# A recurrent attention with two feed-forward layers: four edits to the order of work around the turns of a half batch

## What is computed

```
for t in range(S):
    cur = einsum('bhd,bhe->bhde', u * k[t], v[t])
    y[t] = einsum('bhd,bhde->bhe', r[t], state + cur)
    state = w[t][:, None] * state + einsum('bhd,bhe->bhde', k[t], v[t])
```

## Time and profile before

| | us |
|---|---|
| median of three runs | 777.52 |
| lowest, highest | 776.89, 780.5 |
| the profiled execution's own time | 781.25 |
| its span, first to last instruction | 779.5 |
| TensorE busy | 733.1 (94%) |
| VectorE busy | 475.7 (61%) |
| ScalarE busy | 365.6 (47%) |
| GpSimd busy | 392.9 (50%) |
| mean granted TensorE clock | 0.987 |

### The profile page before, as it was taken

How to read it: one execution, slowest core, us unless ns; L and a number is a source line. 1 busy time by engine, 2 the same in 40 slices (tenths; PEclk the granted TensorE clock), 3 DMA queues, 4 the chain that set the end, 5 groups by cost and what they waited for, 6 DMA issues and landing times.

```text
span 779.5 us, 17757 instructions
## 1 busy us (share of the span) xinstructions
PE 733.1 (94%) x6779; PEld 516.6 (66%) x6779; DVE 475.7 (61%) x967; ACT 365.6 (47%) x735; POOL 392.9 (50%) x372
## 2 busy tenths in 40 slices
PE   4699999999989999999999999998999999999995
PEld 4466656656655665665666666556688878788783
DVE  6998898779666878776787864645333333333331
ACT  3652577656655756746756665542122212212210
POOL 5445488769668869778777876252111111111111
PEclk9998999999999999999999999999999999999998
DMA  9835636365364653645545247994699866766763
GB/s 341 324 150 185 209 132 244 105 241 174 131 238 179 234 215 121 233 165 172 201 142 187 82 162 243 341 345 158 225 383 395 294 245 214 254 237 219 265 222 116
DMA packets 42694, 170.04 MB, mean 218 GB/s; under 512 B 5198, under 2 KB 13136, under 8 KB 37104
## 3 DMA queue, kind: packets, MB, share of 16 engines
q1 hardware_dynamic: 30160, 108.18, 39.1%
q10 hardware_dynamic: 8928, 50.51, 18.5%
q0 software_dynamic: 3520, 10.17, 3.3%
HBM read 132.30 MB, written 37.33 MB: 218 GB/s over the span
## 4 chain that ended last, share of the span: by engine, by line
PE 60%; POOL 9%; DMA 9%; DVE 6%; issue 6%; ACT 3%; SPq 1%; ACTq 0%; POOLq 0%; DVEq 0%
PE bank L1733 5%; PE bank L1876 5%; PE bank L1878 5%; PE bank L1877 5%; PE bank L1735 4%; PE bank L1734 4%; PE bank L1724 4%; PE bank L1722 4%; PE bank L1721 4%; PE bank L1842 4%; PE bank L1844 4%; PE bank L1843 4%; DMA arena<-w_exp_dram 3%; POOL act_buf L606 3%; DMA route_rows<-xrow,pos 2%
## 5 line engine op out<-in xcount | busy, mean ns | idle before, releaser
L606 POOL TENSOR_TENSOR act_buf<-act_buf 128x384 f16<-128x384 f32 x128 | 120.2, 939 | 139.8 <-ACT act_buf L809 138.8
L1291 DVE SCALAR_TENSOR_TENSOR act_buf<-neg,slope,bank 128x384 f32<-128x384 f32 x128 | 77.7, 607 | 92.1 <-ACT neg L802 91.4
L692 POOL DMA_INDIRECT out_dram<-neg,dest x28 | 27.5, 984 | 201.7 <-DVE neg L1560 194.2
L1733 PE MATMUL bank<-arena,act_buf 128*128 128x392 f16 x384 | 127.2, 331 | 1.6 <-ACT xrow L765 1.4
L1721 PE MATMUL bank<-xh,arena 128*128 128x384 f16 x384 | 125.5, 327 | 2.2 <-DVE xl L1093 1.5
L1734 PE MATMUL bank<-arena,act_buf 128*128 128x392 f16 x384 | 127.1, 331 | 0.0
L1735 PE MATMUL bank<-arena,act_buf 128*128 128x392 f16 x384 | 127.0, 331 | 0.0
L1722 PE MATMUL bank<-xl,arena 128*128 128x384 f16 x384 | 125.3, 327 | 0.0
L1842 PE MATMUL bank<-shared,arena 128*128 128x128 f16 x672 | 114.1, 219 | 1.9 <-DVE shared L1486 1.7
L1844 PE MATMUL bank<-shared,arena 128*128 128x128 f16 x672 | 114.1, 219 | 0.0
L1843 PE MATMUL bank<-shared,arena 128*128 128x128 f16 x672 | 114.1, 219 | 0.0
(11 more groups left out here) (185 smaller groups left out, 1563.9 us busy)
## 6 DMA issues: line engine op xcount, KB each, us to landing
arena<-expert_split ACTq DMA_DIRECT2D x28, 1536.0 KB, 7.5
arena<-w_exp_dram SPq DMA_DIRECT2D x32, 768.0 KB, 6.3
expert_split<-arena SPq DMA_DIRECT2D x32, 768.0 KB, 4.7
arena<-expert_split SPq DMA_DIRECT2D x9, 1536.0 KB, 9.2
arena<-rk_in_dram SPq DMA_DIRECT2D x24, 512.0 KB, 6.0
arena<-rk_tok_dram SPq DMA_DIRECT2D x24, 384.0 KB, 3.3
arena<-w_dram SPq DMA_DIRECT2D x24, 256.0 KB, 6.8
shared<-route_rows ACTq DMA_DIRECT2D x31, 197.0 KB, 2.5
```

What stands on the lines that cost most here:

```text
L606: pool.tensor_tensor(gl[:, f % 4, :], gf[:, f % 4, :], gh[:, f % 4, :], ALU.subtract).then_inc(gl_done, 1)
L1733: pe.matmul(at, gh[:, f % 4, ts], woh[:, f, :], start=(f == 0), stop=False)
```

## The change

- VectorE: `y_rows` of the third chunk moves from turn 13 to the end of turn 12, ahead of line 1291 of block 13.
- GpSimd: the third indirect DMA of `scatter` moves from turn 15 to turn 14, and all three now stand ahead of the turn's other work.
- SyncE: `load_w2(0)` moves from the end of the third half's transfers into the middle of the fourth's, ahead of `store_hu(j + 1)` and `load_hu(j + 3)`.
- The multiplication for the tokens between (`inverses`, line 1053) moves for the 20 chunks from the fifth on (m > 3) from VectorE to GpSimd (`inverses_even`), directly ahead of `decayed_k`, and waits for `odd_done` there.

```diff
@@ -457,6 +457,13 @@
             load_rk(1, 0, 2)
             load_tok(1, 0, 2)
 
+            def load_w2(e):
+
+                for i in range(2):
+                    sp.wait_ge(split_out[i], UP + 16 * (2 * e + 2))
+                sp.dma_start(arena[:, w2_at(e):w2_at(e) + 2 * UNIT], wsplit[e][:, 2 * UNIT:4 * UNIT]
+                             ).then_inc(w2_in[e], 16)
+
             def middle(g, j):
                 b, half = g // 2 + 1, g % 2
                 if b < B:
@@ -474,6 +481,9 @@
                 if b < B:
                     load_tok(b, half, 1)
                     load_v(b, half, 1)
+                if g == 3:
+                    sp.wait_ge(wide_free[0], 4)
+                    load_w2(0)
                 store_hu(j + 1)
                 load_hu(j + 3)
                 store_hu(j + 2)
@@ -484,18 +494,8 @@
                     load_rk(b, half, 2)
                     load_tok(b, half, 2)
 
-            def load_w2(e):
-
-                for i in range(2):
-                    sp.wait_ge(split_out[i], UP + 16 * (2 * e + 2))
-                sp.dma_start(arena[:, w2_at(e):w2_at(e) + 2 * UNIT], wsplit[e][:, 2 * UNIT:4 * UNIT]
-                             ).then_inc(w2_in[e], 16)
-
             for g in range(1, 2 * B - 1):
                 middle(g, FIRST_UNIT[g] // 2)
-                if g == 2:
-                    sp.wait_ge(wide_free[0], 4)
-                    load_w2(0)
             sp.wait_ge(khat_done, 6 * B)
             sp.wait_ge(qt_done, 6 * B)
             sp.wait_ge(vl_done, 6 * B)
@@ -547,9 +547,19 @@
             pool.iota(iota_i[:, 32:32 + REST], pattern=[[1, REST]], base=0, channel_multiplier=0
                       ).then_inc(pool_const, 1)
 
+            def inverses_even(m):
+                at = m % 2
+                every_second = inv[:, at, :].rearrange("p (j r) -> p j r", r=2)
+                pool.wait_ge(odd_done, m + 1)
+                pool.tensor_tensor(every_second[:, :, 0], every_second[:, :, 1],
+                                   w_tile(m).rearrange("p (j r) -> p j r", r=2)[:, :, 1], ALU.mult
+                                   ).then_inc(inv_done, 1)
+
             def decayed_k(b, half, c):
 
                 m, at = 6 * b + 3 * half + c, (half + c) % 2
+                if m > NC:
+                    inverses_even(m)
                 pool.wait_ge(inv_done, m + 1)
                 pool.wait_ge(rk_arrived[at], 16 * (3 * b + (3 * half + c) // 2 + 1))
                 if not (isinstance(m, int) and m < NC):
@@ -661,6 +671,8 @@
                                 row_weights(nb, nh, f // 4)
                         if f in lows and not end:
                             unit_low(unit + lows.index(f))
+                        if not start and not end and f in (12, 13, 14):
+                            scatter(g - 1, f - 12)
                         if not last:
                             if f == 11:
                                 decayed_k(b + 1, half, 0)
@@ -673,8 +685,6 @@
                                 decayed_k(b + 1, half, 1)
                             if f == 15:
                                 decayed_q(b + 1, half, 1)
-                        if not start and not end and f in (12, 13, 15):
-                            scatter(g - 1, (12, 13, 15).index(f))
                         if end and f >= 9 and f < 12:
                             scatter(g - 1, f - 9)
 
@@ -1048,6 +1058,8 @@
                 dve.reciprocal(inv[:, at, :].rearrange("p (a j r) -> p a j r", a=NP, r=2)[:, :, :, 1],
                                prod[:, c, :, 1:C + 1].rearrange("p a (j r) -> p a j r", r=2)[:, :, :, 1]
                                ).then_inc(odd_done, 1)
+                if m > NC:
+                    return
                 dve.wait_ge(odd_done, m + 1)
                 every_second = inv[:, at, :].rearrange("p (j r) -> p j r", r=2)
                 dve.tensor_tensor(every_second[:, :, 0], every_second[:, :, 1],
@@ -1322,7 +1334,8 @@
                         if f % 4 == 1 and f > 3:
                             if update(nh, c) and nh + c > 0:
                                 decayed_state(nb, nh, c)
-                            y_rows(nb, nh, c, b_y)
+                            if f < 13:
+                                y_rows(nb, nh, c, b_y)
                             if update(nh, c):
                                 state(nb, nh, c, b_s)
                         if start and f == 6:
@@ -1342,6 +1355,8 @@
                             decays(b + 1, half, 0, b_hid[f][:, 0:C])
                         if f == 12:
                             decays(b + 1, half, 1, b_hid[f][:, 0:C])
+                    if not end and f == 12:
+                        y_rows(nb, nh, 2, b_y)
                     if start and f == 4:
                         w_out_low(0, 1)
                     if start and f in (5, 6):
```

## The result

The changed kernel takes **781.13 us** in the median of 19 runs (775.98 to 786.52), the kernel before 776.89 (771.07 to 780.5, 19 runs): the ratio is 1.006, 95% interval 1.0041 to 1.0078. It is slower by 0.6%, where 770.7 us and "faster" were forecast. Its profiled execution has an own time of 786.03 us and a span of 784.3.

The account below looks back on a forecast made before the run. TensorE was taken to bound the middle halves. Gains of 1.75, 2.5, 0.8 and 1.2 us, 2.5 at the borders, less 2.0 in the fourth half, make 6.8: 777.52 - 6.8 = 770.7 us, range 767.0 to 777.6.

Parts of the forecast that it names:

- The train: GpSimd's work from turn 12 to the end of block 15: 12.1 us, from 10.9.
- the sum: Half by half, TensorE reaches `outputs` of turn 15 by its own work or GpSimd's end, whichever is later; together 6.8 us gained.
- The price of the multiplication: One multiplication of 256 columns on GpSimd takes 0.6 us, from line 606's 0.91 for 384 columns; by section 4.1, 0.85.
- The start of the train: GpSimd's work in each half starts where turn 12 began before; in the fourth half 4.0 us later.
- The step that failed: In turn 1 GpSimd waits for the reciprocal instead of VectorE's slowed multiplication; counted as even.
- The fourth half: W2's load delays ScalarE's expert weights in turn 12 by 4.0 us, to 292.6; the half loses 2.0 us.
- rival 3: W2's load costs its full 9.2 us in the fourth half and the clock drops, 1.7: 777.6 us; chance 0.13.
- Rival 4: GpSimd becomes the bound, its multiplication and VectorE blocking each other, each train 2.7 us longer: 784.2 us; chance 0.07.
- the slack: GpSimd ends at 240.1 in the third half, TensorE takes up `outputs` of turn 15 at 243.80: 3.7 us to spend.
- Rival 2: Part of the gain returns: TensorE waits at block 13, GpSimd's multiplication is disturbed: 773 to 775.5 us; chance 0.17.
- Rival 5: No gain: TensorE's waits are replaced by others of the same sum: 777.5 us; chance 0.05.
- Rival 1: W2's load delays nothing; the fourth half gains 0.8 us instead of losing 2.0: 767.9 us; chance 0.12.

Follow-up runs that it names:

- e10: The changed kernel with turn 14's multiplication left on VectorE, all four parts otherwise in place: 773.95 us, 0.9966 of the kernel before.
- e14: The changed kernel with turn 14's multiplication on VectorE and W2's load behind the second load of expert weights: 769.54 us, 0.9894 of the kernel before.
- e12: The changed kernel with W2's load back and GpSimd's multiplication over tile halves, not every second column: 0.73 us each against 0.84; one execution 770.89 us.
- e13: The changed kernel with VectorE's short gate instructions moved from turn 5 to turn 6, behind `xl`: 776.45 us, 0.9988 of the kernel before.
- e8: The changed kernel with W2's load back, multiplications on GpSimd only from chunk 10 and not in turn 14: 770.49 us, 0.991 of the kernel before.
- e1: The changed kernel with the multiplication back on VectorE; rows, scatter and W2's load as changed: 778.9 us, 1.004 of the kernel before.
- e3: The kernel before with only the rows and the scatter changed: 774.14 us, 0.997 of the kernel before.
- e6: The changed kernel with the multiplication on VectorE and W2's load behind the second load of expert weights: 775.04 us, 0.996 of the kernel before.

## Why the prediction was wrong

**Right.** The waits for `ytok`, `ktok_l`, `att_l` and `xrow` are gone, and the slow clock of the third half with them. The train was given 12.1 us and took 12.5 (228.17 to 240.63), and it does set `outputs` of turn 15 in the third and fifth half, and in the second too, where the sum had TensorE's own work. W2's load was priced at 4.0 us. In e10, where nothing else delays it, ScalarE resumes 45.9 us after the border (286.88 - 241.00) against 41.75 before, 4.1 more; in e14 it is 41.8.

**The price of the multiplication**, 0.6 us, was too low:

```profile
L554 POOL TENSOR_TENSOR arena<-arena x20: 831/842/1156, 65.2 to 436.3; 128x256 f32<-128x256 f32 x20
```

The estimated 0.85 from section 4.1 of the GPSIMD Engine Reference (the Trainium skill) was the right one; the same instruction took 0.43 undisturbed on VectorE. The row of another shape on the same engine, scaled by its columns, was the worse guide; the stride is half of what it was short (0.12 of 0.24, e12). But 0.24 us in a few trains is 1 us of 11.6 (6.8 forecast as gain, 4.8 lost between the two profiled executions).

**The start of the train** was taken from the kernel before. It began 0.5 us later after the border in the third and fifth half and 1.2 in the second (165.68 - 120.24 against 165.97 - 121.68). TensorE waited 1.75, 1.80 and 1.77 us before `outputs` of turn 15 in the second, third and fifth half, where the sum had 0, 1.7 and 0.8: 2.8 us more than forecast, the price above included.

**The step that failed** is "in turn 1 GpSimd now waits for the reciprocal instead of VectorE's slowed multiplication, which I count as even", together with the end of the account at block 15: what comes behind it was put at nothing. In turn 1 GpSimd did not wait. Over all 20 chunks it sat idle for the reciprocal once, for 0.2 us, so the multiplication is 0.83 us of work more there, where 2.31 us of idle time had stood. With that, 0.85 in turn 14, and TensorE earlier by the waits removed, the idle time was used up, and GpSimd ran on to the end of turn 5.

That by itself is not what costs, for in e10 GpSimd runs as long without a wait. What costs is how VectorE enlarges the last 0.85. Against e10, the changed kernel's row sums start 1.0 us later after the border (12.3 against 252.24 - 241.00 = 11.2), and the way from them to `xl` is 1.5 longer, since the short instructions now meet two instructions of GpSimd instead of the gap between them. So `xl` is 2.6 later, all of which TensorE waits, in the fourth and in the sixth half, with the slow clock behind the latter. Those are 1.7 + 5.2 us of the 12.2 between the forecast (6.8 gained) and the middle halves (5.4 lost), and e13 gives back 0.7% (5.6 us) by a mere change of order on VectorE. That they fell on these two halves and not on the third and fifth, where GpSimd runs on as well, is a matter of how the two engines' instructions happen to meet. Only turn 14's multiplication was taken back by itself; what turn 1's alone costs is open.

**The fourth half** was to lose 2.0 and lost 5.1. It has the 2.6 of turn 4, and the clock's 1.7 behind turn 12's wait, which the forecast had put down only for rival 3. ScalarE resumed 6.5 us later than before (292.02 - 243.74 against 41.75), not 4.0. The load was issued 1.9 later after the border, behind the wait before turn 4 (279.56 - 243.74 against 280.74 - 246.84), and took 4.6 longer to land (12.4 against 7.8); e10 does not have that wait, and has 4.1. TensorE's wait there was to be some 2 us for line 616; it was 2.62 for VectorE's block, and 0.3 for line 616.

**The gains were added up as if they were independent.** Rows alone gave 1.001, the scatter 0.997 with them or without, and in e8 they are 0.6%. A wait removed gives nothing while the next one at the same place is as long: `ytok` and `xrow` are two ends of one half, and so are `xrow` and line 616.

**The rivals.** Rival 4 had the sign and the engine, and e8 and e10 bear that out, but neither its mechanism nor its size: the multiplication was not slowed on GpSimd (0.84 in the median, 1.16 at most, against its 3.3), it was VectorE's short instructions that were. It was to decide from 2.0 us per instruction and decided at 0.84, because the slack was taken as 3.7 us up to the border, and what VectorE loses beside GpSimd was left out. Rival 2 named one of the new waits rightly (line 1303, 0.7 us in the third half), rival 3 the clock. Rival 5, other waits in place of the old ones, is what TensorE's waits look like, but their sum is half as much again (14.8 against 9.7). Rival 1, that W2's load delays nothing, fell with e1 against e3 and e6. That the first half counts nothing could not be told from one execution: its slow clock lasts longer in some than in others, with the mean between 0.93 and 0.98 in the profiled executions of these kernels.

## What to carry to other kernels

When work moves to an engine that is half idle, ask not only whether its dense stretch still ends in time, but which idle time behind it had been absorbing lateness, and which short instructions of its neighbour stand between that stretch and a wait. Idle time used up is a warning and not yet a loss (e10 has none and loses nothing by it); it becomes one when the neighbour's instructions no longer meet a gap. Price removed waits together: list for each place what is late next, and expect an edit to look worthless alone that is worth its full size once its neighbours are mended. A prefetch that nobody awaits belongs behind the loads that somebody awaits, in the same queue.

## What the runs showed of the hardware

- VectorE instructions of 0.15 and 0.18 us took 0.95 and 1.70 us, to within 0.05 us the time of GpSimd's instruction beside them, and started with it (257.51 and 257.52; 258.38 and 258.40; in e13 254.20 and 254.21). The Trainium skill's SBUF — State Buffer, section "SBUF: two separate sides", has a rule for it: the shared pair of ports is an exclusive lock between GpSimd and a VectorE instruction with two SBUF inputs or in a two-port mode, held for the whole instruction by whoever starts first, and the other blocks fully. I had drawn on the contention only for instructions of the size that moved. The trace agrees for the comparison, which has two such inputs; in what mode the copy ran no row shows. In proportion the loss was greatest for the shortest instruction: the copy went from 0.15 to 1.69, eleven times, line 1053 from 0.43 to 3.32, eight times. Whether a short one falls into a gap of GpSimd's work, and the 0.09 us in e10 were gap enough, decides between 0.2 and 1.7 us.
- A load of 1536 KB ahead in the same queue delayed the next load, of 768 KB, from 7.8 to 12.4 us.
- Waits of TensorE of the same length did not have the same effect on the clock. Behind 2.62 us in turn 12 (294.82) it stood at 0.50, the 1.2 GHz level, for 3.40 us; behind 2.61 in turn 4 (261.33) it stayed at 1.00. In the sixth half, at the same place in turn 4, 2.64 were followed by 3.40 us at 0.50 again, from 1.2 us behind the wait on:

```profile
294.82:298.22 3.40, 3.40 (x11) 1.60 (x12) 3.25 (x6) 3.37 (x9) 3.22 (x4) 0.50 0.31 109
390.40:393.80 3.40, 3.40 (x13) 1.56 (x12) 2.06 (x4) 1.60 (x3) 0.89 (x1) 0.50 0.92 309
```
